# Filler matmuls ahead of the first projection: fp32r of several widths and quarter tiles in place of fp32

## The chip, the cores and the metric

The kernel runs on one core of one Trainium2 chip. The metric is the time of the whole kernel on the device in microseconds (us). The engines are TensorE (PE; PEld is its weight load), VectorE (DVE), ScalarE (ACT), GpSimd (POOL) and SyncE (SP), which issues all loads and stores.

## What is computed

Three stages in a row, all in float32 at the interface. The first is an attention with a decaying state (4 batches, 8 heads, 768 steps, 48 wide):

```python
state = f[:, :, t, :, None] * state + einsum('bhd,bhe->bhde', k[:, :, t], v[:, :, t])
y[:, :, t] = einsum('bhd,bhde->bhe', q[:, :, t], state)      # f = sigmoid(f_logit)
```

Its result, 3072 rows of 384, goes through an RMS norm and a gated MLP with 1536 hidden columns, `(silu(xn @ w_gate) * (xn @ w_val)) @ w_out`, and then through a second MLP with 2048 hidden columns, `g(x @ w_in) @ w_out`, where g is 0 below -1, the identity above 1 and ((h + 1)^2)/4 between.

## The kernel before

**Tiling.** The 3072 rows are 8 tiles of N = 384 rows (NT = 8), each of 3 blocks of 128 (CT = 3), so 24 blocks n. Attention works by block with the decay in closed form: DVE makes the decays by scans (`decay_after` L689, `decay_upto` L704) and scales k and q (`decay_k` L721, `decay_q` L729); PE transposes the scaled k (`turn_kd`, L299), makes the scores (`score`, L313: 16 matmul records a block, with rows 0 to 63 and 64 to 127 of the array used side by side), the update of the state (`update`, L322) and the output (`attend`, L334 and L338). DVE masks the scores (L748) and adds up the state (L759). ACT sums the squares of the output (L545), POOL makes the reciprocal root (L285, L288), DVE scales the rows into xs (`normalise`, L765), PE transposes xs (`turn_x`, L346), ACT rounds it to fp32r into x_hi (L553) and DVE puts the rest into x_lo (L785).

**Precision.** Projections are done with fp32r operands, each value split in two (hi and lo), as three matmuls for one: hi by hi, hi by lo, lo by hi. So `project` (L399) issues 9 matmuls of 384 columns for a 128-wide part of the hidden columns. Attention, transposes and fillers are fp32 matmuls, and these stand in the trace as two records each (weight load and matmul), while a transpose and an fp32r matmul stand as one.

**Order.** All is written out by hand for each engine; each engine runs its instructions in that order and waits on semaphores. PE does the attention of tile 0 first (`first_attention`, L373), with the fillers in it, then the first MLP of each tile with the attention of the next tile woven in (`gated_mlp`), and then the second MLP. The first projection is `gate(0, 0)` (L508), which waits for x_lo of all three blocks and for the first split weights. DVE has an order of its own for the prologue (L903 to L933), in which the first mask of the scores stands behind the decays of block 1.

**Fillers.** `keep_warm(count)` (L367 to L371) issues matmuls of 128 by 128 weights (ident) and 128 columns (causal) into acc, whose result nobody reads. PE first waits for the six constants that POOL makes (L274 to L282, `consts_ready`) and then for the load of f (`f_loaded`). The counts are WARM_START 10 at the start, WARM_SCORES 6 behind the scores of blocks 0, 1 and 2, WARM_LAST 8 behind the attention of block 2, and WARM_ROWS 3 behind each of the three transposes of xs. POOL's constants are memsets of up to 128 columns and two selects, which wait for four of the memsets.

x_hi and x_lo have two halves, for even and odd tiles. The second half of x_hi (3 x 384 = 1152 columns a partition) is first written by `round_x` for tile 1, during the first MLP of tile 0.

Of the kernel before, what the change touches and what calls it, by code (L numbers as in the profile page):

```python
# [17 lines left out]
F32 = mybir.dt.float32  # L18
# [5 lines left out]
P = 128  # L24

B, H, S, D = 4, 8, 768, 48
# [5 lines left out]
HP = 64  # L32
# [17 lines left out]
WARM_START, WARM_SCORES, WARM_ROWS, WARM_LAST = 10, 6, 3, 8  # L50
# [7 lines left out]
def build(nc, qkf, v, rms_g, wb, wc, out, y_rows):  # L58
    ctx = ExitStack()
    with ctx:  # L60
        def sb(name, shape, dt=F32):
            return ctx.enter_context(nc.sbuf_tensor(name, shape, dt))
# [4 lines left out]
        def sem(name):  # L67
            return ctx.enter_context(nc.semaphore(name))
# [5 lines left out]
        x_hi = sb("x_hi", [P, 2, KM, N], F32R)  # L74
# [31 lines left out]
        causal = sb("causal", [P, C])  # L106
        ident = sb("ident", [P, P])
# [9 lines left out]
        acc = ctx.enter_context(nc.psum_tensor("acc", [P, KM, 512], F32))  # L117
# [3 lines left out]


        consts_ready = sem("consts_ready")
        zeros_ready = sem("zeros_ready")
        g_loaded = sem("g_loaded")
        f_loaded = sem("f_loaded")
# [75 lines left out]
        with nc.Block() as block:  # L202
# [69 lines left out]
            @block.gpsimd  # L272
            def _(pool):
                nc.gpsimd.memset(minus_half[:, :], -0.5).then_inc(consts_ready, 1)  # L274
                nc.gpsimd.memset(eps_col[:, :], EPS).then_inc(consts_ready, 1)
                nc.gpsimd.memset(causal[:, :], 1.0).then_inc(consts_ready, 1)
                nc.gpsimd.memset(ident[:, :], 0.0).then_inc(consts_ready, 1)
                pool.wait_ge(consts_ready, 4)
                nc.gpsimd.affine_select(out=causal[:, :], in_=causal[:, :], compare_op=ALU.is_ge, fill=0.0,
                                        base=0, pattern=[[1, C]], channel_multiplier=-1).then_inc(consts_ready, 1)  # L280
                nc.gpsimd.affine_select(out=ident[:, :], in_=ident[:, :], compare_op=ALU.not_equal, fill=1.0,
                                        base=0, pattern=[[-1, P]], channel_multiplier=1).then_inc(consts_ready, 1)  # L282
                with pool.Fori(0, NCH) as n:
                    pool.wait_ge(ssq_ready, n + 1)
                    nc.gpsimd.tensor_tensor(mean[:, :], ssq[:, :], eps_col[:, :], ALU.add)\  # L285
                        .then_inc(mean_ready, 1)
                    pool.wait_ge(mean_ready, n + 1)
                    nc.gpsimd.tensor_tensor(rstd[:, :], mean[:, :], minus_half[:, :], ALU.pow)\  # L288
                        .then_inc(rstd_ready, 1)
# [3 lines left out]
            def _(pe):  # L293
                def turn_kd(n, c):
                    pe.wait_ge(kd_ready, n + 1)
                    if not isinstance(n, int) or n > 0:
                        pe.wait_ge(scores_ready, 2 * n)
                    for p in range(NP):
                        mm = pe.transpose(ta[:, p * PR:(p + 1) * PR], kd[0:PR, c % 2, p, :], ident[0:PR, 0:PR])  # L299
                    mm.then_inc(kdT_made, 1)  # L300

                def score(n, c, first=False):

                    pe.wait_ge(qd_ready, n + 1)
                    if first and n > 0:
                        pe.wait_ge(state_ready, n)
                    if not first:
                        pe.wait_ge(x_lo_ready, n)
                    pe.wait_ge(kdT_ready, n + 1)
                    for p in range(NP):  # L310
                        for r, t in enumerate((tb, ta)):
                            rows = slice(r * HP, (r + 1) * HP)
                            mm = pe.matmul(t[:, p * C:(p + 1) * C], kd[rows, c % 2, p, :], qd[rows, c % 2, p, :],  # L313
                                           start=True, stop=True)
                    mm.then_inc(scores_made, 1)

                def update(n):
                    pe.wait_ge(v_loaded, 16 * (n + 1))
                    pe.wait_ge(kdT_ready, n + 1)
                    pe.wait_ge(scores_ready, 2 * n + 1)  # L320
                    for p in range(NP):
                        mm = pe.matmul(tb[0:PR, p * 2 * D:(p + 1) * 2 * D], kdT[:, p, :],  # L322
                                       v_sb[:, :, p, :], start=True, stop=True)
                    mm.then_inc(update_made, 1)

                def attend(n, c, half):
                    if half == 0:
                        pe.wait_ge(scores_ready, n * 2 + 2)
                        pe.wait_ge(decayed_ready, n + 1)
                        if not isinstance(n, int) or n > 0:  # L330
                            pe.wait_ge(xs_ready, n)
                    for p in range(half * NP // 2, (half + 1) * NP // 2):
                        o = p * 2 * D
                        pe.matmul(y_ps[:, o:o + 2 * D], qd[0:PR, c % 2, p, :], decayed[0:PR, p, :],  # L334
                                  start=True, stop=False, skip_group_check=True)
                        for r in range(2):
                            h = slice(o + r * D, o + (r + 1) * D)
                            mm = pe.matmul(y_ps[:, h], scores[:, r, p, :], v_sb[:, r, p, :],  # L338
                                           start=False, stop=True, skip_group_check=True)
                    mm.then_inc(y_made, 1)  # L340

                def turn_x(n, bank=tb):
                    pe.wait_ge(xs_ready, n + 1)
                    pe.wait_ge(state_ready, n + 1)
                    for k in range(KM):
                        mm = pe.transpose(bank[:, k * P:(k + 1) * P], xs[:, k * P:(k + 1) * P], ident[:, :])  # L346
                    mm.then_inc(xT_made, 1)
# [16 lines left out]
                        elif o == 13:  # L364
                            turn_x(n)

                def keep_warm(count):  # L367


                    for _ in range(count):  # L370
                        pe.matmul(acc[:, 0, 0:P], ident[:, :], causal[:, :], start=True, stop=True)  # L371

                def first_attention():  # L373

                    pe.wait_ge(f_loaded, 16)
                    keep_warm(WARM_START)
                    turn_kd(0, 0)
                    score(0, 0, True)
                    keep_warm(WARM_SCORES)
                    for n in range(CT):  # L380
                        update(n)
                        attend(n, n, 0)
                        if n + 1 < CT:
                            turn_kd(n + 1, n + 1)
                        attend(n, n, 1)
                        if n + 1 < CT:
                            score(n + 1, n + 1, True)
                            keep_warm(WARM_SCORES)
                        else:
                            keep_warm(WARM_LAST)  # L390
                        turn_x(n, (gate_ps, val_ps)[n % 2])
                        keep_warm(WARM_ROWS)

                def project(i, j, part, bank):

# [109 lines left out]
                pe.sem_inc(out2_made, 1)  # L505
                pe.wait_ge(consts_ready, 6)
                first_attention()
                gate(0, 0)  # L508
                gated_mlp(0, 1)
# [728 lines left out]
```

## Time and profile before

| what | us |
| --- | --- |
| median of 3 runs | 1015.99 |
| lowest and highest run | 1015.89, 1016.22 |
| profiled execution: span, first to last instruction | 1013.9 |
| PE busy in it | 1000.9 (99%) |
| DVE, ACT, POOL busy | 586.5, 342.7, 19.5 |
| first projection (L399) starts | 37.20 |

The profile is of one execution. Its own time as a run isn't given apart from the three runs shown; the median of these is 2.1 us above the span, which counts from the first to the last instruction only. Times in rows are us from the start of the span, durations us, unless they say ns. A timeline row gives the start of a group, its length from the start of the first record to the end of the last, the engine, line, operation, output and inputs, and how many records it merges; in brackets the idle time of the engine before it and what ended it. A row of a table by stretches gives the stretch, its length, the busy us (and records) of PE, PEld, DVE, ACT and POOL, then the granted clock of TensorE as a share of full speed, the busy share of the DMA engines, and GB/s. Records overlap: a matmul's duration is longer than the step to the next one.

### The profile page before, as it was taken

The page shows a single profiled execution, that of the slowest core. Times are in us where ns is not written, and L with a number is a line of the kernel's source. Part 1 is how long each engine was busy: PE and PEld are TensorE (multiplying, and loading weights), DVE is VectorE, ACT ScalarE, POOL GpSimd, SP SyncE. Part 2 cuts the span into 40 slices and gives each one's busy share as a digit, 9 for nine tenths or more (in the row PEclk, how much of TensorE's full clock was granted, in tenths as well). Part 3 has the DMA queues.
Part 4 walks back from the last instruction along what each step waited for, and adds up shares of the span by engine and source line. Part 5 has one row for each costly group of instructions (what it writes and reads, how often), then busy time and mean ns, then how long its engine had stood idle before and what let it go on. Part 6 is the DMA issues. An engine that isn't in the chain of part 4 may idle for free.

```text
span 1013.9 us, 16822 instructions
## 1 busy us (share of the span) xinstructions
PE 1000.9 (99%) x6307; PEld 985.1 (97%) x6307; DVE 586.5 (58%) x1196; ACT 342.7 (34%) x624; POOL 19.5 (2%) x58
## 2 busy tenths in 40 slices
PE   7999999999999999999999999999999999999998
PEld 7899999999999999999999999999999999999998
DVE  8777564665565664664663665545554545454553
ACT  2343322322322322222222444344344443434343
POOL 0000000000000000000000000000000000000000
PEclk9999999999999999999999999999999999999999
DMA  5541111111111011111121230000000000000000
GB/s 187 185 143 40 40 39 41 39 39 47 31 46 39 31 47 39 39 39 39 39 68 48 80 92 2 1 23 0 23 0 23 0 23 0 23 0 23 0 24 24
DMA packets 15768, 42.22 MB, mean 42 GB/s; under 512 B 1408, under 2 KB 8064, under 8 KB 15744
## 3 DMA queue, kind: packets, MB, share of 16 engines
q1 hardware_dynamic: 15744, 41.88, 12.3%
q8 instruction: 17, 0.28, 0.1%
q14 instruction: 7, 0.06, 0.0%
HBM read 37.16 MB, written 4.72 MB: 41 GB/s over the span
## 4 chain that ended last, share of the span: by engine, by line
PE 93%; DVE 4%; issue 1%; POOL 1%; ACT 0%; DMA 0%; POOLq 0%; DVEq 0%
PE gate_ps L399 14%; PE val_ps L399 14%; PE acc L475 13%; PE gate_ps L463 10%; PE val_ps L463 10%; PE acc L421 9%; PE acc L479 7%; PE acc L425 5%; PE y_ps L338 4%; PE tb L313 2%; PE y_ps L334 2%; PE tb L322 2%; DVE qd L717 1%; PE ta L299 1%; DVE kd L726 1%
## 5 line engine op out<-in xcount | busy, mean ns | idle before, releaser
L833 DVE TENSOR_TENSOR h_lo<-h_buf,h_hi 128x384 fp32r<-128x384 f32 x224 | 123.2, 550 | 13.2 <-ACT h_hi L644 6.2
L475 PE MATMUL acc<-h_hi,w_hi 128*128 128x384 f32 x381 | 127.5, 335 | 0.0
L475 PE MATMUL acc<-h_hi,w_lo 128*128 128x384 f32 x381 | 127.3, 334 | 0.0
L637 ACT ACTIVATE act_buf<-act_buf,half_col 128x384 f32<-128x384 f32 x128 | 78.7, 615 | 140.4 <-DVE act_buf L883 140.4
L580 ACT ACTIVATE act_buf<-gate_ps 128x384 f32<-128x384 f32 x96 | 47.2, 491 | 180.9 <-PE gate_ps L399 180.9
L399 PE MATMUL gate_ps<-x_hi,w_hi 128*128 (+1 forms) x288 | 100.5, 349 | 2.0 <-DVE h_buf L822 1.5
L585 ACT ACTIVATE h_hi<-h_buf 128x384 fp32r<-128x384 f32 x96 | 50.4, 525 | 151.0 <-DVE h_buf L828 151.0
L421 PE MATMUL acc<-h_hi,w_hi 128*128 128x384 f32 x288 | 100.4, 349 | 0.0
L399 PE MATMUL val_ps<-x_hi,w_hi 128*128 (+1 forms) x288 | 100.2, 348 | 0.0
L399 PE MATMUL gate_ps<-x_hi,w_lo 128*128 (+1 forms) x288 | 96.7, 336 | 0.0
L421 PE MATMUL acc<-h_hi,w_lo 128*128 128x384 f32 x288 | 96.6, 335 | 0.0
L399 PE MATMUL gate_ps<-x_lo,w_hi 128*128 (+1 forms) x288 | 96.6, 335 | 0.0
L399 PE MATMUL val_ps<-x_hi,w_lo 128*128 (+1 forms) x288 | 96.6, 335 | 0.0
L399 PE MATMUL val_ps<-x_lo,w_hi 128*128 (+1 forms) x288 | 96.5, 335 | 0.0
L644 ACT ACTIVATE h_hi<-h_buf 128x384 fp32r<-128x384 f32 x128 | 67.2, 525 | 80.4 <-DVE h_buf L888 80.4
L822 DVE TENSOR_TENSOR h_buf<-gate_ps,act_buf 128x384 f32<-128x384 f32 x96 | 53.0, 552 | 68.1 <-ACT act_buf L580 67.9
L479 PE MATMUL acc<-h_lo,w_hi 128*128 128x384 f32 x381 | 86.5, 334 | 0.0
L828 DVE TENSOR_TENSOR h_buf<-val_ps,h_buf 128x384 f32<-128x384 f32 x96 | 53.5, 557 | 52.7 <-PE val_ps L399 51.1
L883 DVE TENSOR_SCALAR act_buf<-val_ps 128x384 f32<-128x384 f32 x64 | 35.6, 556 | 66.9 <-PE val_ps L463 66.9
L475 PEld LDWEIGHTS acc<-h_hi,w_hi 128*128 128x128 f32 x381 | 71.5, 188 | 0.6
L475 PEld LDWEIGHTS acc<-h_hi,w_lo 128*128 128x128 f32 x381 | 71.5, 188 | 0.0
L479 PEld LDWEIGHTS acc<-h_lo,w_hi 128*128 128x128 f32 x381 | 67.9, 188 | 0.0
(117 smaller groups left out, 2040.5 us busy)
## 6 DMA issues: line engine op xcount, KB each, us to landing
raw<-qkf_dram SPq DMA_DIRECT2D x21, 768.0 KB, 4.3
x<-wb_dram SPq DMA_DIRECT2D x12, 576.0 KB, 5.9
v_sb<-v_dram SPq DMA_DIRECT2D x24, 192.0 KB, 2.8
out_dram<-x SPq DMA_DIRECT2D x7, 576.0 KB, 2.8
raw<-wc_dram SPq DMA_DIRECT2D x7, 384.0 KB, 3.1
x<-qkf_dram SPq DMA_DIRECT2D x2, 768.0 KB, 6.5
kd<-wc_dram SPq DMA_DIRECT2D x3, 384.0 KB, 3.2
qd<-wc_dram SPq DMA_DIRECT2D x3, 384.0 KB, 3.4
```

What stands on the lines that cost most here:

```text
L399: mm = pe.matmul(bank[:, 0:N], wb_part(w, j, part, k), x[:, par, k, :], start=(k == 0 and x is x_hi and w is w_hi), stop=(k == KM - 1 and ...
L421: pe.matmul(acc[:, m, 0:N], wb_part(w, j, 2, m), h_hi[:, j % 2, :], start=(j == 0 and w is w_hi), stop=False)
L425: mm = pe.matmul(acc[:, m, 0:N], wb_part(w_hi, j, 2, m), h_lo[:, j % 2, :], start=False, stop=(j == JB - 1))
L463: mm = pe.matmul(t[:, 0:N], wc_part(w, j, 0, k), x[:, i % 2, k, :], start=(k == 0 and x is x_hi and w is w_hi), stop=(k == KM - 1 and w is ...
L475: pe.matmul(acc[:, m, 0:N], wc_part(w, j, 1, m), h_hi[:, j % 2, :], start=(j == 0 and w is w_hi), stop=False)
L479: mm = pe.matmul(acc[:, m, 0:N], wc_part(w_hi, j, 1, m), h_lo[:, j % 2, :], start=False, stop=(j == JC - 1))
L585: nc.scalar.activation(h_hi[:, j % 2, :], h_buf[:, j % 2, :], ACT.Copy).then_inc(h_hi_ready, 1)
L637: nc.scalar.activation(act_buf[:, j % 2, :], act_buf[:, j % 2, :], ACT.Square, bias=half_col[:, :], scale=0.5).then_inc(square_ready, 1)
L644: nc.scalar.activation(h_hi[:, j % 2, :], h_buf[:, j % 2, :], ACT.Copy)\
L822: nc.vector.tensor_tensor(h_buf[:, j % 2, :], gate_ps[:, 0:N], act_buf[:, 0, :], ALU.mult)\
L828: nc.vector.tensor_tensor(h_buf[:, j % 2, :], val_ps[:, 0:N], h_buf[:, j % 2, :], ALU.mult)\
L833: nc.vector.tensor_tensor(h_lo[:, j % 2, :], h_buf[:, j % 2, :], h_hi[:, j % 2, :].bitcast(F32), ALU.subtract).then_inc(done, 1)
```

## The change

The fillers become four kinds. `keep_warm(count, columns)` now multiplies a part of x_hi's second half, as fp32r, by itself: weights are its first 128 columns, and the moving operand its first `columns` columns. `keep_warm_tiles(count)` issues, count times over, four fp32 matmuls, one for each quarter of the array: 64 rows, 64 weight columns, 48 moving columns (D), the two row halves into different banks of acc and the two column halves into different partitions. POOL fills x_hi's second half with 1.0 ahead of its two selects, and PE waits for that (`warm_ready`) before the first filler.

| place | before | after |
| --- | --- | --- |
| start | 10 fp32, 128 columns | 10 fp32r, 512 columns |
| behind the scores of block 0 | 6 fp32, 128 | 12 fp32r, 256 |
| behind the scores of blocks 1 and 2 | 6 fp32, 128 | 3 rounds of 4 quarter tiles, fp32, 48 |
| behind the attention of block 2 | 8 fp32, 128 | 16 fp32r, 128 |
| behind each transpose of xs | 3 fp32, 128 | 6 fp32r, 384 |

```diff
+        warm_ready = sem("warm_ready")
...
                 nc.gpsimd.memset(ident[:, :], 0.0).then_inc(consts_ready, 1)
+                nc.gpsimd.memset(x_hi[:, 1, :, :].bitcast(F32), 1.0).then_inc(warm_ready, 1)
                 pool.wait_ge(consts_ready, 4)
...
-                def keep_warm(count):
-
+                warm = x_hi[:, 1, :, :].rearrange("p k n -> p (k n)")
+
+                def keep_warm(count, columns):
 
                     for _ in range(count):
-                        pe.matmul(acc[:, 0, 0:P], ident[:, :], causal[:, :], start=True, stop=True)
+                        pe.matmul(acc[:, 0, 0:columns], warm[:, 0:P], warm[:, 0:columns], start=True, stop=True)
+
+                def keep_warm_tiles(count):
+
+                    for _ in range(count):
+                        for r in range(2):
+                            for c in range(2):
+                                pe.matmul(acc[c * HP:(c + 1) * HP, 1 + r, 0:D], ident[r * HP:(r + 1) * HP, 0:HP],
+                                          causal[r * HP:(r + 1) * HP, 0:D], start=True, stop=True)
 
                 def first_attention():
 
                     pe.wait_ge(f_loaded, 16)
-                    keep_warm(WARM_START)
+                    pe.wait_ge(warm_ready, 1)
+                    keep_warm(WARM_START, 512)
                     turn_kd(0, 0)
                     score(0, 0, True)
-                    keep_warm(WARM_SCORES)
+                    keep_warm(2 * WARM_SCORES, 256)
                     for n in range(CT):
                         update(n)
                         attend(n, n, 0)
...
                             score(n + 1, n + 1, True)
-                            keep_warm(WARM_SCORES)
+                            keep_warm_tiles(WARM_SCORES // 2)
                         else:
-                            keep_warm(WARM_LAST)
+                            keep_warm(2 * WARM_LAST, 128)
                         turn_x(n, (gate_ps, val_ps)[n % 2])
-                        keep_warm(WARM_ROWS)
+                        keep_warm(2 * WARM_ROWS, 384)
```

## Rows read from the trace of the kernel before

**Rows 1.** The page: busy times, and the chain that ended last by engine.

```profile
PE 1000.9 (99%) x6307; PEld 985.1 (97%) x6307; DVE 586.5 (58%) x1196; ACT 342.7 (34%) x624; POOL 19.5 (2%) x58
...
PE 93%; DVE 4%; issue 1%; POOL 1%; ACT 0%; DMA 0%; POOLq 0%; DVEq 0%
```

**Rows 2.** Busy time by stretch with granted clock.

```profile
3.55:13.20 9.65, 8.05 (x52) 7.45 (x53) 8.68 (x26) 2.35 (x4) 0.00 (x0) 1.00 0.98 348
...
20.80:28.40 7.60, 7.60 (x75) 7.42 (x76) 6.50 (x11) 2.67 (x5) 0.74 (x2) 1.00 0.22 71
...
37.20:1012.00 974.80, 970.92 (x6052) 956.75 (x6052) 557.49 (x1128) 331.37 (x604) 15.72 (x42) 1.00 0.11 35
```

**Rows 3.** Timeline from 3 to 15 us, PE and DVE.

```profile
3.58 4.60 PE L371 MATMUL acc<-causal,ident 128*128 128x128 f32 x20 [3.58 <-DMA raw<-qkf_dram]
...
10.43 0.27 PE L313 MATMUL ta<-qd,kd 64*128 64x128 f32 x1
...
10.54 0.27 PE L313 MATMUL ta<-qd,kd 64*128 64x128 f32 x1
...
12.41 0.67 DVE L748 TENSOR_TENSOR scores<-tb,causal 128x512 f32<-128x512 f32 x1
...
14.56 0.57 PE L338 MATMUL y_ps<-v_sb,scores 128*128 128x48 f32 x4
...
14.96 0.43 PE L334 MATMUL y_ps<-decayed,qd 112*128 112x96 f32 x2
```

**Rows 4.** The chain that ended last, 20 to 29 us: start, length, what.

```profile
20.80 0.55 PE gate_ps L346 x3
21.34 0.67 PE acc L371 x6
...
26.86 1.53 PE acc L371 x12
```

**Rows 5.** Timeline, fillers behind the scores of blocks 1 and 2, and xs.

```profile
18.51 1.60 PE L371 MATMUL acc<-causal,ident 128*128 128x128 f32 x12
...
26.79 1.60 PE L371 MATMUL acc<-causal,ident 128*128 128x128 f32 x12
...
27.32 0.62 DVE L765 SCALAR_TENSOR_TENSOR xs<-y_ps,rstd,g_rows 128x384 f32<-128x384 f32 x1 [0.73 <-POOL rstd L288]
...
28.23 0.49 PE L346 MATMUL val_ps<-ident,xs 128*128 128x128 f32 x3
```

**Rows 6.** Timeline, the end of the prologue, PE and DVE.

```profile
32.64 2.02 PE L371 MATMUL acc<-causal,ident 128*128 128x128 f32 x16
...
34.76 0.62 DVE L765 SCALAR_TENSOR_TENSOR xs<-y_ps,rstd,g_rows 128x384 f32<-128x384 f32 x1 [0.71 <-POOL rstd L288]
...
35.82 0.83 PE L371 MATMUL acc<-causal,ident 128*128 128x128 f32 x6
37.20 0.41 PE L399 MATMUL gate_ps<-x_hi,w_hi 128*128 128x384 f32 x1 [0.55 <-issue]
```

**Rows 7.** Timeline, fp32r matmuls of 384 columns, nine steps apart.

```profile
37.80 0.33 PE L399 MATMUL gate_ps<-x_hi,w_hi 128*128 128x384 f32 x1
...
39.36 0.33 PE L399 MATMUL val_ps<-x_hi,w_hi 128*128 128x384 f32 x1
```

**Rows 8.** Durations in ns, min/median/max: to 9 us, all, and 7 to 10 us.

```profile
L371 PE MATMUL acc<-causal,ident x20: 421/421/551, 3.6 to 7.8; 128*128 128x128 f32 x20
...
L371 PE MATMUL acc<-causal,ident x90: 275/275/551, 3.6 to 36.4; 128*128 128x128 f32 x90
...
L299 PE MATMUL ta<-ident,kd x4: 394/394/394, 8.0 to 8.5; 112*128 112x112 f32 x4
```

**Rows 9.** Timeline of POOL to 2 us.

```profile
0.88 0.20 POOL L276 MEMSET causal<- 128x128 f32 x1
1.02 0.20 POOL L277 MEMSET ident<- 128x128 f32 x1
...
1.54 0.29 POOL L281 TENSOR_SCALAR_AFFINE_SELECT ident<-ident 128x128 f32<-128x128 f32 x1
```

## The prediction

> **What bounds the kernel now.** I read the page first, to see where the time lies. TensorE (PE) is busy for 99% of the span, in all forty slices, and the chain of work that ended last runs through it for 93%; the filler matmuls that the change touches, L371, are not among the costly groups [rows 1]. A table by stretches then cuts the span where the first projection begins: of 974.8 us behind 37.20 us PE is busy in 970.9 [rows 2]. Nothing there is edited, so what the change is worth is how much later or earlier the first projection starts. All fillers lie ahead of it: 45 matmuls, 90 records [rows 8].
>
> The timeline tells which fillers stand in someone's way. Ahead of 13.2 us the bound is VectorE (DVE), not PE: the 16 score matmuls are issued by 10.54 us, but the mask that reads them starts at 12.41, when DVE is through with work of its own; the transposes L299, which wait behind the ten start fillers, have that same cover [rows 3]. So about 12.41 − (10.54 + 0.27) = 1.6 us of PE delay is free there. From 20.80 to 32.6 us the chain stands on PE, which is busy in all of the 7.60 us to 28.40 [rows 2]: transposes of block 0, fillers L371 x6, updates, attention, scores, fillers x12, transposes of block 1, fillers x6, updates [rows 4]. The twelve at 26.79 matter by a hair: the xs that the next transposes need is ready at 27.32 + 0.62 = 27.94, the transposes start at 28.23 [rows 4, 5]. The last sixteen (32.64 to 34.66) end before xs of block 2 (34.76 + 0.62 = 35.38), and the last six (from 35.82) leave 0.55 us of idle before the projection, which by the code waits for x_lo, at 37.20 [rows 6]. The twelve of block 0 (18.51 to 20.11) end well before the transposes behind them, which start at 20.80 [rows 4, 5].
>
> **Prices.** Each fp32 filler is two records. Twelve records take 1.60 us with a last one of 0.275 (the median of the 90) [rows 5, 8], so a record costs (1.60 − 0.275)/11 = 0.120 us and a filler 0.24. An fp32r matmul of 384 columns is one record; nine steps from 37.80 to 39.36 make 0.173 us each [rows 7].
>
> Start fillers, 10 of 512 columns. The column of granted clock shows 1.00 here [rows 2], but the records don't: L371 takes a median 421 ns here against 275 over all of its records, and the four transposes behind it are as long, 394 [rows 8], where the scores show 0.27 us at 10.43 [rows 3]. I read that as TensorE at its lower level (1.2 GHz) until at least 8.5 us and at the upper one (2.4 GHz) by the scores. Twenty records took (4.60 − 0.421)/19 = 0.220 each, 4.4 us in all. By proportion 512 columns cost 0.173 × 512/384 = 0.231 at the upper level, times 0.220/0.120 = 0.42 at the lower one: 4.2 us. Change −0.2 to 0, under the 1.6 us of cover: 0.
>
> The first scores' fillers, 12 of 256 columns: by proportion 0.115, by the fp32 record 0.120; 1.4 us as before. They end at about 12.2, and the updates wait for DVE's mask until 13.08: 0.
>
> The fillers behind each xs transpose (three places), 6 of 384 columns for 3 of fp32: 6 × (0.173 − 0.120) = +0.32 us. At blocks 0 and 1 this is on the chain at full price: +0.32 twice. At the third, the idle of 0.55 us in front of the projection covers it: 0, with 0.2 us of cover left.
>
> The quarter tiles, 3 rounds of 4 matmuls, 48 columns, 64 rows and 64 weight columns, fp32, so 24 records (two places). No row shows one. The nearest is L313, two row halves side by side with 128 weight columns: two records every 0.11 us, 0.055 each [rows 3]. Below, if halved weight columns halve it: 24 × 0.0275 = 0.66 us. Above, if tiles run one by one at the pace of L338 (48 columns, full array: four records from 14.56 to 14.96, 0.10 each): 24 × 0.10 = 2.4 us [rows 3]. I take L313's pace, 1.3 us, since it too splits the array. At block 0 they end at 18.51 + 1.3 = 19.8, before xs: 0. At block 1 they start 0.32 late, at 27.11, end at 28.43, and xs is there at 28.26: the transposes move from 28.23 to 28.43, so the delay by then is 0.20 instead of 0.32 (the tiles are shorter and give 0.12 back, and no more than about 0.25 can be had, as xs binds next). With the fillers behind them: 0.20 + 0.32 = 0.52. The ends: 0.39 with short tiles; with serial ones +0.1 at block 0, then 0.1 + 0.32 = 0.42, tiles from 27.2 to 29.6, transposes +1.4, and 1.7 in all.
> The Trainium skill ("TensorE: Matmul & The Clock Gate", Part 3, on packing) says that tiles in different rows and columns of the array run concurrently; by it the four matmuls of a round would cost about as one, the lower end above, and the sum would be 0.4 instead of 0.52. No row here shows column tiles.
>
> The last fillers, 16 of 128 columns for 8 of fp32. The stream alone would be 16 × 0.058 = 0.9 us, but weights are loaded for each, and no row with 128 weight columns over the full array steps faster than L338's 0.10; I take 0.12, 1.9 us as before. Above: an fp32r matmul of this narrow shape costs what the fp32 one of the same shape costs, 0.24, 3.8 us. By the former they end at 33.2 + 1.9 = 35.1 with xs at 35.90: 0. By the latter at 37.0: +1.0.
>
> The memset of 1152 columns on POOL goes ahead of the two selects, and PE waits for both the memset and the selects. 128 columns take 0.14 us from start to start [rows 9]: at most 0.0011 us a column, 1.3 us. The selects then end near 1.54 + 0.29 + 1.3 = 3.1, and PE starts its first filler at 3.58, on a DMA [rows 3, 9]: 0, with 0.4 us of cover and the 1.6 us of DVE's cover behind that. SP's queue is not touched, though its loads of v and w for blocks 1 to 3 are issued on y_made by the code and move with the chain.
>
> **Sum:** 0.32 + (−0.12) + 0.32 = +0.52 us on a span of 1013.9. The median of the three runs is 1015.99, about 2.1 above the span; I put that unchanged on top: 1015.99 + 0.52 = 1016.5. Behind 37.20 everything follows PE and should move as one. About 0.2% (2.0 us) is what a measurement of this kernel can tell from no change.
>
> **Rivals.**
> A. The quarter tiles run one after another, and packing doesn't do what it is written for. For it: y_ps matmuls of 48 columns don't get cheaper than 0.10 though they have few columns, so small matmuls are bound by something else than columns. Against: L313's halves do overlap. Price +1.7: 1017.7. Chance 0.10.
> B. The narrow fp32r fillers cost like fp32. For it: no row has an fp32r matmul under 384 columns. Against: nothing in the 384-column rows hints at a second pass. They take the place of xs of block 2 as what the transposes wait for: 0.52 + 1.0 = +1.5, 1017.5. Chance 0.06.
> C. The other side, slower: the granted clock. The place is the stretch of quarter tiles (18.5 or 26.8 us), where a shorter, smaller load and a longer idle (from 19.8 to 20.8 instead of from 20.1) stand for dense full-array fillers; or the start, where the clock rises later on fp32r ones. PE needed from 3.58 to at least 8.5, at most 10.4 us [rows 3, 8], so 5 to 7 us, to get the upper level the first time; a fall at 27 us costs by the middle of these 6 × (1 − 0.120/0.220) = 2.7 us, all of it on the chain. 0.52 + 2.7 = 3.2: 1019.2. It decides as soon as one fall occurs between 20.8 and 33 us; a late rise alone has 1.6 us of cover. Against it: the fillers at 26.79, behind a stretch of 48- to 112-column matmuls, still show the upper level's 0.120 [rows 5], and the body behind 37.20, mostly fp32r matmuls, holds 1.00 [rows 2]. Chance 0.06; with A and B together, or a longer clock fall, 0.04 more above 1018.
> D. Filler is filler: what PE gains or loses is taken up by waits and the time stays within 0.1 us of before, 1016.0. Against: the chain has no gap at 21 and 28 us. Chance 0.06.
> E. Faster by over 0.2% would need more than 2 us out of a prologue of which the fillers on the chain hold 0.67 + 1.53 + 0.67 = 2.9 us, all of which stay in some form. Chance 0.02.
>
> **How the numbers follow.** The forecast holds 0.66, D 0.06, A 0.10, B 0.06, C 0.06, the combinations 0.04, E 0.02. Range: from 1015.8 (D, less the runs' own spread of 0.1) to 1017.9 (A with the spread); it leaves out C, the combinations, E and the edges. Faster 0.02; slower 0.10 (C and the combinations); same 0.88.
>
> **What would show it.** In the profile of the changed kernel: start fillers near 0.42 us a step, ending at or before 8 us; scores' mask still at 12.4; twelve 256-column records in 1.4 to 1.5 us; six of 384 columns in 1.04 at three places; 24 small records in 1.3 us, twice, with PE idle before the transposes of block 0; the sixteen narrow ones in 1.9 us with PE idle behind them; the first gate matmul at 37.7 instead of 37.20. Record durations of 275 ns growing to 400 or more behind 10 us would be C; transposes of block 2 that wait for fillers and not for xs would be B; a tile stretch of over 2 us would be A. I am wrong if the first gate matmul moves by less than 0.2 or more than 1 us, or if the stretch behind it changes length.

## The result, and the profile after

Over 20 runs of each kernel the median went from 1015.84 us to 1017.75; the ratio is 1.0017 with a 95% interval of 1.0009 to 1.0025. The lowest runs are 1015.48 and 1016.25. What stands out is the spread. Of the kernel before 18 of 20 runs lie between 1015.48 and 1016.22 and two are higher (1018.08 and 1019.77). Of the changed one 8 lie between 1016.25 and 1016.97, eight between 1017.65 and 1018.21, one at 1018.93 and three above 1020. The profiled run is one of the low ones: 1016.50 us, span 1014.8 against 1013.9.

Timeline of PE in the changed kernel, to be held against [rows 3], [rows 5] and [rows 6]. L374 is now the fp32r filler, L381 the quarter tiles, L348 the transpose of xs, L411 the projection.

```profile
3.64 3.85 PE L374 MATMUL acc<-x_hi 128*128 128x512 f32 x10 [3.64 <-DMA raw<-qkf_dram]
...
10.39 1.69 PE L374 MATMUL acc<-x_hi 128*128 128x256 f32 x12
13.34 1.00 PE L324 MATMUL tb<-v_sb,kdT 128*112 128x96 f32 x8 [1.27 <-DVE scores L760]
...
18.62 0.56 PE L381 MATMUL acc<-causal,ident 64*64 64x48 f32 x24
20.91 0.55 PE L348 MATMUL gate_ps<-ident,xs 128*128 128x128 f32 x3 [1.72 <-DVE xs L777]
21.21 1.32 PE L374 MATMUL acc<-x_hi 128*128 128x384 f32 x6
22.36 0.93 PE L324 MATMUL tb<-v_sb,kdT 128*112 128x96 f32 x8
...
27.31 0.56 PE L381 MATMUL acc<-causal,ident 64*64 64x48 f32 x24
28.52 0.55 PE L348 MATMUL val_ps<-ident,xs 128*128 128x128 f32 x3 [0.64 <-DVE xs L777]
...
33.37 1.98 PE L374 MATMUL acc<-x_hi 128*128 128x128 f32 x16
36.18 0.55 PE L348 MATMUL gate_ps<-ident,xs 128*128 128x128 f32 x3 [0.83 <-DVE xs L777]
36.48 1.29 PE L374 MATMUL acc<-x_hi 128*128 128x384 f32 x6
37.95 0.41 PE L411 MATMUL gate_ps<-x_hi,w_hi 128*128 128x384 f32 x1 [0.18 <-issue]
```

The projection starts at 37.95 instead of 37.20. The tiles take 0.56 us where six fp32 fillers took 1.60, so PE now idles 1.72 us in front of the transposes of block 0, and 0.64 in front of those of block 1, where it did not wait before. In the chain that ended last, the fillers behind both transposes are 1.07 us long, against 0.67 and 0.67 [rows 4]:

```profile
21.45 1.07 PE acc L374 x6
...
29.07 1.07 PE acc L374 x6
```

Behind the start of the projection next to nothing changed. The row of the table by stretches, with the same 6052 records, has PE busy for 970.96 of 974.95 us, where [rows 2] have 970.92 of 974.80.

```profile
37.95:1012.90 974.95, 970.96 (x6052) 956.68 (x6052) 557.73 (x1128) 331.40 (x604) 15.78 (x42) 1.00 0.10 35
```

So this profile explains a span longer by 0.9 us (0.75 ahead of the projection, 0.15 behind), near the +0.8 between the lowest runs. It doesn't show where the median's +1.9 comes from. The experiments look for that. Each kernel ran 12 times, each set of four kernels beside 35 runs of the kernel before on the same chip. The three sets ran on three chips, so a comparison across sets is weaker than one with the kernel before of the same set. The span of each run is the figure to go by; "high" below means a span over 0.9 us above the lowest of the same kernel and set.

| kernel | lowest / median span | median us | high runs |
| --- | --- | --- | --- |
| before, three sets | 1014.1 / 1014.3; 1014.0 / 1014.2; 1013.8 / 1014.0 | 1016.25; 1016.11; 1015.78 | 6, 9 and 8 of 35 |
| changed (the 20 runs above) | 1014.6 / 1016.15 | 1017.75 | 12 of 20 |
| changed, again | 1014.7 / 1016.1 | 1017.74 | 7 of 12 |
| tiles alone | 1014.0 / 1015.9 | 1017.98 | 10 of 12 |
| tiles undone | 1014.6 / 1014.9 | 1016.80 | 5 of 12 |
| start alone | 1013.8 / 1014.1 | 1015.97 | 1 of 12 |
| tiles long | 1014.2 / 1014.4 | 1016.25 | 1 of 12 |
| short dense | 1013.9 / 1014.0 | 1015.73 | 4 of 12 |
| last alone | 1014.0 / 1014.5 | 1016.23 | 4 of 12 |
| both undone | 1014.7 / 1014.9 | 1016.67 | 0 of 12 |
| steady | 1013.9 / 1014.05 | 1015.67 | 1 of 12 |
| lean | 1013.2 / 1013.35 | 1015.08 | 0 of 12 |
| changed, filled | 1014.6 / 1014.8 | 1016.54 | 3 of 12 |
| rows alone | 1014.7 / 1014.8 | 1016.52 | 2 of 12 |

Each run also has a mean granted clock. Of the 23 high runs of the kernel before 21 have 0.995 or 0.996, and two (1016.0 and 1016.2) have 1.000, for which no profile shows the cause. The limit on the span misses some falls: three runs of the changed kernel at 1015.0 to 1015.2 have 0.997 and 0.998, as its high ones do. Counted by a mean clock of 0.998 or less it is 25 of 105 for the kernel before, 15 of 20 and 10 of 12 for the changed one, 5 for last alone and 0 for changed, filled; the other rows keep their count.

### The profile page after: what moved, and what is told of

Read it like the earlier page. It is cut to its first block, busy times and chain, and to the rows that moved or that the text cites. A ratio compares the mean times of both kernels' runs of the same rounds, so it can differ in the third digit from the quotient of the medians.

```text
span 1014.8 us, 16851 instructions
## 1 busy us (share of the span) xinstructions
PE 999.2 (98%) x6321; PEld 982.5 (97%) x6321; DVE 586.7 (58%) x1196; ACT 342.7 (34%) x624; POOL 20.6 (2%) x59
## 4 chain that ended last, share of the span: by engine, by line
PE 93%; DVE 4%; issue 1%; POOL 1%; ACT 0%; DMA 0%; POOLq 0%; DVEq 0%
PE gate_ps L411 14%; PE val_ps L411 14%; PE acc L487 13%; PE gate_ps L475 10%; PE val_ps L475 10%; PE acc L433 9%; PE acc L491 7%; PE acc L437 5%; PE y_ps L340 4%; PE y_ps L336 2%; PE tb L315 2%; PE tb L324 2%; DVE qd L729 1%; PE ta L301 1%; DVE kd L738 1%
## 5 line engine op out<-in xcount | busy, mean ns | idle before, releaser
L411 PE MATMUL gate_ps<-x_hi,w_hi 128*128 (+1 forms) x288 | 100.5, 349 | 1.7 <-DVE h_buf L834 1.5
L411 PE MATMUL val_ps<-x_hi,w_hi 128*128 (+1 forms) x288 | 100.2, 348 | 0.0
L411 PE MATMUL val_ps<-x_hi,w_lo 128*128 (+1 forms) x288 | 96.6, 336 | 0.0
L411 PE MATMUL gate_ps<-x_hi,w_lo 128*128 (+1 forms) x288 | 96.6, 335 | 0.0
L411 PE MATMUL val_ps<-x_lo,w_hi 128*128 (+1 forms) x288 | 96.5, 335 | 0.0
L411 PE MATMUL gate_ps<-x_lo,w_hi 128*128 (+1 forms) x288 | 96.5, 335 | 0.0
```

The source lines that it names most:

```text
L411: mm = pe.matmul(bank[:, 0:N], wb_part(w, j, part, k), x[:, par, k, :], start=(k == 0 and x is x_hi and w is w_hi), stop=(k == KM - 1 and ...
```

## The experiments

### First set: which part scatters

**The changed kernel again**, no edit.

> The changed kernel once more, for more runs and a second profile. Theory T (tiles): the quarter tiles weigh so little on the array that in some runs the granted clock drops to its lower level around 18 to 21 us; runs scatter from 1016.3 to about 1020.9, those of clock 0.999 or more at 1016.3 to 1016.6, those of 0.998 at 1017 to 1018, those of 0.995 and less above 1018.5. Theory S (start): the fp32r start fillers let the clock rise too late in some runs; same scatter. Theory W (widths alone): no clock effect, 1016.6 with 0.3 us of scatter; then the scatter seen was chance.

The scatter came again: spans from 1014.7 to 1020.5, with mean clocks from 0.999 down to 0.992, and the profiled run (span 1017.6) shows the cause. Table by stretches of that run; the column behind POOL's is the granted clock:

```profile
20.00:22.00 2.00, 1.08 (x5) 1.08 (x6) 1.97 (x5) 0.26 (x1) 0.00 (x0) 0.77 0.73 280
22.00:25.00 3.00, 3.00 (x17) 2.98 (x16) 0.75 (x3) 1.28 (x2) 0.00 (x0) 0.58 0.00 2
25.00:28.00 3.00, 3.00 (x29) 2.95 (x30) 2.92 (x5) 0.64 (x2) 0.00 (x0) 1.00 0.00 0
...
38.00:40.00 2.00, 2.00 (x9) 2.00 (x8) 0.56 (x1) 0.49 (x1) 0.00 (x0) 0.54 0.99 278
40.00:42.00 2.00, 2.00 (x9) 2.00 (x9) 0.00 (x0) 0.00 (x0) 0.00 (x0) 0.61 0.60 226
```

The clock fell to 0.5 (1.2 of 2.4 GHz) twice: once behind the idle that follows the first tiles, and once behind the wait that follows the sixteen narrow fillers. Between 22 and 25 us PE is "busy" all the time, yet the six wide fillers that start at 21.36 us take 2.27 us, where the changed kernel's first profile has 1.32. The projection starts at 40.04, 2.84 us later than in [rows 6]. Theory W falls.

**Tiles alone.**

```diff
                             score(n + 1, n + 1, True)
-                            keep_warm(WARM_SCORES)
+                            keep_warm_tiles(WARM_SCORES // 2)
```

> The kernel before with only the quarter tiles put in behind the scores of blocks 1 and 2; all other fillers stay fp32. Sum of the terms without a clock effect: -0.25 us (xs of block 1 binds), 1015.6. Theory T: scatter as in the changed kernel, several runs 1 to 4 us above the lowest, clock 0.998 and less in them. Theory S: tight, within 0.4 us, near 1015.6.

Ten of 12 runs are high, against 6 of 35 of the kernel before beside them. The two lowest (1014.0, 1014.1) are no longer than that kernel's lowest: without a fall the tiles cost nothing, and save 0.1 us if anything. The profiled run has a span of 1019.5. First its table by stretches, then its timeline of PE:

```profile
18.60:19.20 0.60, 0.60 (x28) 0.44 (x24) 0.57 (x2) 0.00 (x0) 0.56 (x1) 1.00 0.27 32
19.20:20.90 1.70, 0.02 (x4) 0.00 (x0) 1.67 (x5) 0.00 (x0) 0.00 (x0) 1.00 0.75 172
20.90:21.90 1.00, 0.96 (x9) 0.96 (x10) 1.00 (x2) 0.37 (x1) 0.00 (x0) 1.00 0.88 326
21.90:35.60 13.70, 13.70 (x96) 13.29 (x95) 6.38 (x11) 4.77 (x8) 0.75 (x2) 0.50 0.36 125
35.60:42.80 7.20, 5.89 (x51) 5.51 (x50) 4.98 (x7) 1.20 (x4) 1.15 (x2) 1.00 0.86 294
```

```profile
18.66 0.56 PE L378 MATMUL acc<-causal,ident 64*64 64x48 f32 x24
20.94 0.55 PE L346 MATMUL gate_ps<-ident,xs 128*128 128x128 f32 x3 [1.72 <-DVE xs L773]
...
42.82 0.41 PE L407 MATMUL gate_ps<-x_hi,w_hi 128*128 128x384 f32 x1 [0.55 <-issue]
```

The clock fell 1 us after PE had resumed from 1.7 us of idle, and stayed low for 13.7 us although PE was busy throughout. The projection started at 42.82, 5.6 us later than in [rows 6]. Theory T stands, S falls for this kernel.

**Tiles undone.** The changed kernel with the six fp32 fillers back in these two places.

```diff
-                            keep_warm_tiles(WARM_SCORES // 2)
+                            keep_warm_fp32(WARM_SCORES)
```

> The changed kernel with the six fp32 fillers back in the two places of the quarter tiles. Without a clock effect +0.80 us from the wider fillers behind both transposes: 1016.6. Theory T: tight, within 0.4 us, all clocks 0.999 or more. Theory S: scatter as in the changed kernel, up to 1020.

The median span came to 1014.9, and none reaches 1017, but the kernel isn't tight: five runs lie at 1015.9 to 1016.5. The profiled one (1015.9) has one fall, at 36.7 us. Stretches, then timeline:

```profile
35.50:36.40 0.90, 0.07 (x2) 0.02 (x1) 0.62 (x1) 0.00 (x0) 0.17 (x1) 1.00 0.97 358
...
36.70:40.10 3.40, 3.40 (x14) 3.40 (x12) 0.56 (x1) 0.49 (x1) 0.00 (x0) 0.50 0.79 292
```

```profile
36.38 0.65 PE L348 MATMUL gate_ps<-ident,xs 128*128 128x128 f32 x3 [0.83 <-DVE xs L782]
36.69 2.27 PE L374 MATMUL acc<-x_hi 128*128 128x384 f32 x6
38.75 0.52 PE L416 MATMUL gate_ps<-x_hi,w_hi 128*128 128x384 f32 x1
```

Here the six fillers behind the last transposes, 1.29 us at the upper level, last 2.27 and hold up the projection, which starts at 38.75 with records of 520 ns. Theory T doesn't cover this; there is a second place.

**Start alone.** The kernel before with the memset, the wait for it and `keep_warm_fp32r(WARM_START, 512)`.

> The kernel before with only the ten start fillers as fp32r of 512 columns, and the memset for them. Without a clock effect no change, 1015.8. Theory T: tight, 1015.8. Theory S: scatter, some runs at 1017 to 1020.

Tight but for one run of 12 at 1018.0, no more than the kernel before has (6 of 35). The start is not what scatters.

### Second set: idle or light load

**Tiles long and short dense.** The tiles are shorter than the fillers they replace, and lighter. These kernels keep one of the two each; both are edits of the kernel before.

```diff
-                            keep_warm(WARM_SCORES)
+                            keep_warm_tiles(2 * WARM_SCORES)
```

```diff
-                            keep_warm(WARM_SCORES)
+                            keep_warm(WARM_SCORES // 3)
```

> The kernel before with twelve rounds of quarter tiles in place of three behind the scores of blocks 1 and 2: 96 records at a step of 0.015 us, 1.4 us, as long as the six fp32 fillers, so PE idles no longer than before (0.7 us at block 0). Theory I (idle): the clock falls because PE idles for 1.7 us at block 0; then this kernel is as tight as the kernel before, spans at 1014.2. Theory L (light load): quarter-array matmuls of 48 columns don't hold the clock, however many; then it scatters as with three rounds, most spans 1.5 to 5 us above the lowest.

> The kernel before with two fp32 fillers in place of six behind the scores of blocks 1 and 2: 0.5 us, about as long as the three rounds of tiles, but full array; PE idles about 1.8 us at block 0. Theory I: scatter as with the tiles (median span near 1015.9, several at 1017 and above). Theory L: tight, median 1014.0, since xs of block 1 binds 0.25 us earlier.

Tiles long has one high run of 12, and its lowest is 0.2 us above that of the kernel before: quarter tiles for as long as the old fillers are as good as these in this count. So light load alone isn't the cause. Short dense keeps the long idle, as its timeline shows:

```profile
18.75 0.71 PE L371 MATMUL acc<-causal,ident 128*128 128x128 f32 x4
21.04 0.55 PE L346 MATMUL gate_ps<-ident,xs 128*128 128x128 f32 x3 [1.57 <-DVE xs L765]
```

Four of its runs are high (1015.3 to 1017.2), eight are not. That is less than the ten of the tiles with nearly the same idle, and with 9 of 35 in the kernel before beside them 4 of 12 isn't told from chance. So neither theory holds as it was put. What the three kernels show together: short and light (tiles alone, first set) is high in 10 of 12; long and light in 1; short and dense in 4. With these tiles it takes the idle, and what stands around it seems to weigh too. How much each weighs 12 runs can't say.

The one high run of tiles long was the profiled one, and it shows something about the kernel before. Its code up to 18 us is that kernel's:

```profile
12.10:13.30 1.20, 0.16 (x3) 0.04 (x1) 1.20 (x4) 0.00 (x0) 0.00 (x0) 1.00 0.98 403
13.30:15.30 2.00, 1.93 (x17) 1.80 (x17) 1.99 (x5) 0.00 (x0) 0.00 (x0) 1.00 0.10 41
15.30:25.60 10.30, 10.30 (x141) 9.89 (x140) 7.01 (x18) 1.68 (x5) 0.78 (x2) 0.50 0.23 80
```

The clock fell at 15.3 us, behind the wait for DVE's mask (1.04 us) and a stretch of attention matmuls, and stayed low for 10.3 us. The span was 1018.2 with a mean clock of 0.995, like the 13 of 105 runs of the kernel before that lie between 1017.7 and 1018.1, all with 0.995. Last alone was profiled in such a run too, with the fall at 15.0 us.

**Last alone.** The kernel before with sixteen fp32r fillers of 128 columns for the eight fp32 ones behind the attention of block 2.

> The kernel before with only the last fillers (behind the attention of block 2) as sixteen fp32r of 128 columns. They last as long as the fp32 ones (1.98 against 2.02 us). Theory N (narrow fp32r is a light load for its time): a third to a half of the runs have the clock fall near 36 us and are 1.0 to 1.8 us longer: spans 1014.2 and 1015.5. Theory W (the wider fillers or something else in the changed kernel causes those falls): tight, 1014.2.

Four high runs: 1015.3, 1016.7, 1017.8 and 1018.0. Two of these are of the kind just seen. That leaves two, too few to tell from the kernel before. Inconclusive by itself.

**Both undone.** The changed kernel with fp32 fillers in both suspect places.

> The changed kernel with fp32 fillers back behind the scores of blocks 1 and 2 and behind the attention of block 2. Left of the change: the start (512 columns), the 256 columns behind the scores of block 0, the 384 columns behind each transpose. Theory N with L or I: tight at the median span 1014.2 + 0.8 = 1015.0, no group of runs at 1016. Theory W: a third of the runs at 1016 as with only the tiles undone.

No high run, spans from 1014.7 to 1015.3, median +0.7 over the kernel before in its set (1014.2). Against tiles undone (5 of 12 high, another set and chip), the only difference in the kernel is the sixteen narrow fillers. With the fall at 36.7 us in one profile and that at 38 in another, theory N is likely, but 5 against 0 of 12 is thin. That these fillers take 1.98 us against 2.02, with the same wait behind them (0.83 against 0.78 us), says that here it would be the weight and not the idle. And the length of an idle isn't all elsewhere either: in front of the first updates this kernel's profile has 1.31 us of idle and that of the kernel before 0.87, yet none of these 12 runs is of the kind that falls at 15 us.

### Third set: filling the idle

**Steady.** The kernel before with more of its own fillers where PE waits.

```diff
                     score(0, 0, True)
-                    keep_warm(WARM_SCORES)
+                    keep_warm(9)
...
-                            keep_warm(WARM_SCORES)
+                            keep_warm((8, WARM_SCORES)[n])
                         else:
-                            keep_warm(WARM_LAST)
+                            keep_warm(10)
```

> The kernel before with more of its own fp32 fillers where PE waits anyway: 9 for 6 behind the scores of block 0, 8 for 6 behind those of block 1, 10 for 8 behind the attention of block 2. Each addition lies under a wait of 0.7 to 0.9 us, so nothing moves on the path. Theory I (a clock fall begins in an idle of PE, more often the longer and the lighter the work around it): all twelve runs within 0.5 us, span 1014.2, no run at 1016 to 1018 as the kernel before has in a fifth of its runs. Rival (falls come from outside the fillers, at random): one fifth of the runs stay at 1016 to 1018.

Nothing above 1014.9, where the kernel before had eight of 35 at 1016.2 to 1018.0. Nine runs lie at 1013.9 to 1014.1, three at 1014.8 and 1014.9; so "within 0.5 us" was too narrow. No run at 1016 or above in 12, against 8 in 35, is thin by itself; with lean below it is none in 24.

**Changed, filled.**

```diff
-                    keep_warm(2 * WARM_SCORES, 256)
+                    keep_warm(3 * WARM_SCORES, 256)
...
-                            keep_warm_tiles(WARM_SCORES // 2)
+                            keep_warm_tiles((14, 8)[n])
                         else:
-                            keep_warm(2 * WARM_LAST, 128)
+                            keep_warm(22, 128)
```

> The changed kernel with more of its own fillers in the idle stretches: 18 for 12 of 256 columns, 14 and 8 for 3 and 3 rounds of quarter tiles, 22 for 16 of 128 columns. Theory I: tight at the span of the changed kernel without falls, 1014.8 to 1015.0; the kinds of filler are then not to blame, only their length. Theory L (light load): quarter tiles and narrow fp32r don't hold the clock, half of the runs stay at 1016 and above.

The median drops from the changed kernel's 1017.7 (on other chips) to 1016.54, with nothing above 1015.7 in span and no mean clock below 0.999. Tiles and narrow fillers are not to blame by their kind alone: with their idle filled no run shows a fall. Three runs are at 1015.6 to 1015.7, and the profiled one tells of a third way to lose: timeline, and the durations (ns, min/median/max) of the fillers behind the scores of block 0.

```profile
11.74 3.07 PE L374 MATMUL acc<-x_hi 128*128 128x256 f32 x18
14.65 0.93 PE L324 MATMUL tb<-v_sb,kdT 128*112 128x96 f32 x8
```

```profile
L374 PE MATMUL acc<-x_hi x18: 278/283/580, 11.7 to 14.5; 128*128 128x256 f32 x18
```

The clock rose late: the fillers begin at 11.74 instead of 10.39, the first of them are up to 580 ns long instead of 283, and the last ends at 14.8, past the first mask of DVE (12.53 to 13.19). The updates start at 14.65 instead of 13.34: more filler than a late rise leaves room for costs about 1 us. All three runs have a mean clock of 1.000, since the column counts 1.00 ahead of the first rise. Those of steady near 1014.8 have 0.999, 0.999 and 0.998, so one at least looks like a fall instead; no profile shows it.

**Lean**, as steady, and without fillers where PE has real work at once.

```diff
-                            keep_warm(WARM_SCORES)
+                            keep_warm((8, 4)[n])
...
-                        keep_warm(WARM_ROWS)
+                        if n == CT - 1:
+                            keep_warm(WARM_ROWS)
```

> As steady, but with no fillers behind the transposes of xs of blocks 0 and 1, and 4 in place of 6 behind the scores of block 1: there PE has real work at once, and the fillers stand on the chain. Saving: about 0.5 at block 0 (the mask of the scores, ready at 21.34, binds next), 0.25 in front of the transposes of block 1 and 0.67 behind them: 1.4 us, span 1012.8. Theory I: tight too, since PE idles nowhere longer than 0.3 us more. Rival: the fillers behind the transposes are what holds the clock; then falls near 21 and 28 us bring runs at 1015 and above.

The fastest and tightest of all: 12 spans from 1013.2 to 1013.5, median 1015.08 us against 1015.78, ratio 0.9989 (0.9980 to 0.9997). The gain on undisturbed runs is 0.65 us, not the 1.4 expected. Its timeline against [rows 4] and [rows 5]:

```profile
20.88 0.55 PE L346 MATMUL gate_ps<-ident,xs 128*128 128x128 f32 x3 [0.23 <-DVE xs L766]
21.57 1.00 PE L322 MATMUL tb<-v_sb,kdT 128*112 128x96 f32 x8
...
27.78 0.55 PE L346 MATMUL val_ps<-ident,xs 128*128 128x128 f32 x3
28.47 1.00 PE L322 MATMUL tb<-v_sb,kdT 128*112 128x96 f32 x8
...
36.50 0.41 PE L400 MATMUL gate_ps<-x_hi,w_hi 128*128 128x384 f32 x1 [0.55 <-issue]
```

From the start of the transposes to the updates 0.69 us pass in both places, where the kernel before has 1.05 and 1.00. In the chain that ended last DVE's mask now stands there (20.83 to 21.43 and 27.64 to 28.33), so the updates wait for it, and of the 0.67 us of fillers on the chain about half came back. At block 1 the expectation had left that wait out.

**Rows alone.** The kernel before with six fp32r fillers of 384 columns for three fp32 ones behind each transpose.

> The kernel before with only the fillers behind the three transposes of xs changed: six fp32r of 384 columns for three fp32. The profile of the changed kernel has them at 1.07 us on the chain against 0.67, twice: +0.8 us, span 1015.0 in undisturbed runs. No longer idle anywhere, so no more falls than the kernel before (a fifth of the runs). Rival: the wider fillers raise the clock's falls; more than a third of the runs above 1016.

Lowest 1014.7 against 1013.8, median span 1014.8 against 1014.0: +0.8 to +0.9 as expected, and two of 12 high. That is as much as the changed kernel's lowest runs are above those of the kernel before, and it is no sign of more falls (8 of 35 in the kernel before).

## Why the prediction was right or wrong

The range (1015.8 to 1017.9) holds 1017.75 and the direction was right: slower, under 0.2%. That is in good part luck. The middle, 1016.5, is right only for a run without a clock fall. The median was made by rival C, falls of the clock, which the forecast priced at 1019.2, gave a chance of 0.06 and left out of its range; the upper end is that of rival A, which the profile refutes. By its own sign (wrong if the first gate matmul moves by more than 1 us) the forecast held in the first profile, +0.75, and failed in the second of the same kernel, +2.84.

**Sum on the path.** Forecast +0.52, and the first projection moved by 0.75; 0.11 of it is DVE's start, whose mask begins at 12.52 instead of 12.41, since the load that starts the chain ended 0.11 later (3.55 instead of 3.44). Of the terms, "+0.32 twice" was too small: the chain has 1.07 − 0.67 = +0.40 twice. The tiles "give 0.12 back", it said; it was 0.2: 28.23 + 0.11 + 0.40 would be 28.74, and the transposes start at 28.52, on xs, which the forecast had named as the next bound. 0.40 − 0.22 + 0.40 + 0.11 = 0.69 of 0.75. Of the rest, 0.05 lies at block 1: from the start of the transposes to the updates it has 1.45 us for 1.00, where block 0 has 1.45 for 1.05. On undisturbed runs the kernel with both suspects undone gives +0.7 and rows alone +0.8.

**Quarter tiles.** "I take L313's pace, 1.3 us" failed, and so did the lower bound of 0.66. They take 0.56, (0.56 − 0.218)/23 = 0.015 us a record, the last one being 218 ns long:

```profile
L381 PE MATMUL acc<-causal,ident x48: 218/218/253, 18.6 to 27.7; 64*64 64x48 f32 x48
```

That is rival A refuted: 24 records take 0.56 us and not 2.4. It agrees with what the Trainium skill ("TensorE: Matmul & The Clock Gate", Part 3) says, that matmuls in different tiles of the array run concurrently; no run puts all four on one quarter, so how much the side by side gives isn't shown. By that rule the tiles would have been booked nearer (0.66 us, and 0.25 given back, against 0.56 and 0.22), but the sum, 0.4, would have been farther from 0.75 than 0.52 was, since the undersized fillers and the later load had no part in it. On the price: the two records of an fp32 matmul are not a weight load and a matmul, as was said ahead of the prediction; ten fillers stand as 20 matmul records and 20 of weight load. The mistake that mattered was another: short was booked as a small gain (0.12 us) and a 1 us idle, and came as 1.72 us of idle.

**Prices that held.** Narrow fillers: 1.98 us for 16 (forecast 1.9), not the 3.8 of rival B; they don't bind. The 256-column ones: 1.69 against 1.4 to 1.5, under cover. The start: 3.85 us against 4.2, under DVE's cover, and start alone is unchanged. It is shorter because the clock rose within it (records of 387 to 763 ns, and transposes of 258 ns behind, against 394 in [rows 8]); where it stayed low, in changed, filled, the ten took 4.61 us. Of the six profiles with these start fillers four have it up when the transposes start, by 7.8 us, and one not before 11.7. The memset took 1.06 us (bound 1.3), the last select ended at 2.81, and PE still started on the DMA. DVE's cover held: mask at 12.5. The idle before the projection took in the third set of wide fillers, with 0.18 us left of 0.55 (forecast 0.2).

**Rival C.** The place was named (the stretch of quarter tiles, with its shorter and smaller load and longer idle), and the price of 2.7 us lies between what was seen: +1.5 to 2 in most high runs, 5.6 in the worst profile, since the clock stayed low for 3.4 us in one fall and 13.7 in another. The chance was too small. It leaned on "the fillers at 26.79 … still show the upper level" and the main body's 1.00, that is on one execution, and on three runs within 0.3 us. A fall is an event of single runs: the kernel before has it in a fifth of them (23 of 105), which three runs miss half the time (0.78 cubed is 0.48). One quiet profile says little on that.

**D and E** didn't happen.

## What to carry to other kernels

Judge fillers that hold TensorE's clock first by how much of each wait they fill: count the idle behind them in the profile, and extend them up to it, but not beyond what stays hidden if the clock rises late. The light kinds went without a fall here when they were long enough (0 of 12 in changed, filled); whether dense ones forgive a longer idle is open (4 of 12 high against 10 of 12). Where PE has real work next, a filler stands on the path and costs its length. An effect that comes in some runs only can be missed by a profile and by three runs; ask for the span and the mean clock of a dozen runs before giving it a small chance.

## What the runs showed of the hardware

The clock fell to 1.2 GHz 2.0 us after PE had resumed from an idle of 1.04 us (tiles long), 1.0 and 0.2 us after idles of 1.72 and 1.73 (tiles alone; changed, again), and 0.3 us after one of 0.83 that followed narrow fillers (tiles undone). Once low it stayed so for 10.3 us (tiles long), 13.7 (tiles alone) and 3.4 (changed, again, at 21 us, and tiles undone) with PE's busy share at 100%. The two long stretches held attention matmuls of 48 to 128 columns and fillers of as few, the short ones wide fillers too; what decides the length isn't shown. So a busy row is no sign of an upper clock; the length of a like record is: eight updates take 1.67 us low (tiles alone) and 0.93 high. The first rise, with PE at work from about 3.6 us, came as early as in the start fillers (by 7.3 us, changed) and once later than 11.7 (changed, filled). The table by stretches shows a granted clock of 1.00 ahead of the first rise though the matmuls there take 421 ns for 275 [rows 8]. Four quarter tiles in fp32, 48 columns wide, cost 0.12 us together (8 records of 0.015), as much as one of the two records of a full fp32 matmul of 128 columns [rows 5].
